# The opening of the convolution stage: nested branches, six PSUM banks, high and low parts first, two stores by SyncE

## The reference

```python
scores = 0.125 * q @ k.T            # 8 heads of 64: window 32, or window 32 with dilation 4
x = softmax(where(mask, scores, -1e9)) @ v
e = argmax(x @ w_gate)              # or the expert before, where sigmoid(x @ w_local) >= 0.5
y = p[e] * (relu(x @ w1[e]) @ w2[e])            # 8 experts, 512 -> 1024 -> 512
gate = sigmoid(sum_k conv_w[k] * y[t - 4 + k])  # 5 taps along the sequence, per channel
out = (gate * (y @ w_val)) @ w_out
```

## Time and profile before

| | before |
|---|---|
| median of 3 runs | 598.66 us (597.76 to 599.15) |
| the profiled execution, its own time | 595.05 us |
| its span in the profile | 593.3 us |
| PE busy | 544.3 us (92%) |
| DVE busy | 267.0 us (45%) |
| ACT busy | 216.0 us (36%) |
| POOL busy | 257.3 us (43%) |
| instruction fetch of PE (queue q8) | 34 packets, 0.56 MB |

### The profile page before, as it was taken

One profiled execution on the slowest core, in us unless ns is written; L12 is line 12 of the kernel. 1 busy time (PEld: TensorE's weight loads), 2 busy tenths in 40 slices (PEclk: granted clock), 3 DMA queues, 4 the chain that ended last, 5 costly groups with the idle time before them and its releaser, 6 DMA issues.

```text
span 593.3 us, 10062 instructions
## 1 busy us (share of the span) xinstructions
PE 544.3 (92%) x3274; PEld 461.8 (78%) x3274; DVE 267.0 (45%) x858; ACT 216.0 (36%) x503; POOL 257.3 (43%) x161
## 2 busy tenths in 40 slices
PE   7899999973779999999999999999899586999997
PEld 3789988862568888888888887888688486999986
DVE  4677777755821121312222121122112689998710
ACT  2677777741021221212212121121112555565421
POOL 1000010471168475937275559674953445621210
PEclk9999999995889999999999999999999589999999
DMA  5849499959079996996889797979681522211012
GB/s 170 248 131 265 106 271 315 285 184 288 21 220 372 327 371 210 373 320 244 269 289 312 256 347 221 398 246 382 230 272 51 148 63 66 90 50 54 36 72 88
DMA packets 62772, 128.42 MB, mean 216 GB/s; under 512 B 9664, under 2 KB 17856, under 8 KB 62208
## 3 DMA queue, kind: packets, MB, share of 16 engines
q1 hardware_dynamic: 38560, 68.43, 35.7%
q0 software_dynamic: 17392, 46.93, 24.6%
q10 hardware_dynamic: 6768, 12.36, 6.0%
HBM read 104.28 MB, written 23.41 MB: 215 GB/s over the span
## 4 chain that ended last, share of the span: by engine, by line
PE 56%; DMA 21%; DVE 8%; POOL 6%; issue 5%; SPq 3%; ACT 1%; PEldq 0%; POOLq 0%; ACTq 0%; DVEq 0%
PE bank L1159 39%; DMA stage<-in_moe_w 10%; PE bank L1176 5%; POOL w_low L564 5%; PE bank L1197 4%; DMA w_high<-in_moe_w 3%; DMA dil_logits<-lg_dil 2%; PE bank L1185 2%; PE bank L1312 2%; DVE gate_acc L971 2%; DMA kT<-in_k 2%; DMA stage<-in_moe_w_val 1%; PE bank L1220 1%; DMA vwin<-in_v 1%; PE bank L1375 1%
## 5 line engine op out<-in xcount | busy, mean ns | idle before, releaser
L564 POOL TENSOR_TENSOR w_low<-stage,w_high 128x2048 fp32r<-128x2048 f32 x32 | 146.8, 4595 | 82.3 <-DMA stage<-in_moe_w 59.0
L1159 PE MATMUL bank<-w_high,x_high 128*128 x184 | 74.7, 406 | 5.7 <-POOL w_low L564 3.1
L1014 ACT ACTIVATE probs<-shifted,negmax 96x128 f32<-96x128 f32 x192 | 66.4, 394 | 35.7 <-PE bank L1185 22.1
L1159 PE MATMUL bank<-w_high,h_high 128*128 x184 | 74.2, 403 | 1.4 <-POOL w_low L564 1.4
L917 DVE TENSOR_TENSOR x_low<-bank,x_high 128x512 fp32r<-128x512 f32 x25 | 17.3, 691 | 127.1 <-ACT x_high L1055 127.1
L1159 PE MATMUL bank<-w_high,x_low 128*128 x184 | 72.6, 394 | 0.0
L1159 PE MATMUL bank<-w_low,x_high 128*128 x184 | 72.1, 392 | 0.0
L1159 PE MATMUL bank<-w_high,h_low 128*128 x184 | 72.1, 392 | 0.0
L1159 PE MATMUL bank<-w_low,h_high 128*128 x184 | 71.7, 390 | 0.0
L1055 ACT CAST x_high<-bank 128x512 fp32r<-128x512 f32 x25 | 14.7, 588 | 152.5 <-PE bank L1283 152.5
L553 POOL DMA_DIRECT2D w_high<-in_moe_w x32 | 24.2, 767 | 101.7 <-DVE x_dil L739 83.4
(11 more groups left out here) (184 smaller groups left out, 1054.5 us busy)
## 6 DMA issues: line engine op xcount, KB each, us to landing
w_high<-in_moe_w POOLq DMA_DIRECT2D x32, 1024.0 KB, 12.8
stage<-in_moe_w SPq DMA_DIRECT2D x32, 1024.0 KB, 7.9
y_sorted<-y_sb ACTq DMA_DIRECT2D x25, 256.0 KB, 7.4
vwin<-in_v SPq DMA_DIRECT2D x4, 1560.0 KB, 7.4
x_sorted<-gathered SPq DMA_DIRECT2D x21, 256.0 KB, 8.2
x_in<-x_sorted ACTq DMA_DIRECT2D x21, 256.0 KB, 5.6
kT<-in_k SPq DMA_DIRECT2D x32, 152.0 KB, 4.7
out<-o_sb SPq DMA_DIRECT2D x18, 256.0 KB, 2.0
```

The lines of the kernel that those rows point to most:

```text
L564: g.tensor_tensor(low, stage[:, c % 2, :], high.bitcast(F32), ALU.subtract).then_inc(split_done, 1)
L1014: a.activation(probs[:, j % 2, u, :], shifted[:, j % 2, u, :], ACT.Exp, bias=negmax[:, j % 2, u:u + 1], scale=-1.0).then_inc(exp_done, 1)
L1159: ins = mm(dst, l, r, start=first and i == 0, stop=last and i == 2)
```

## The change

- PE: the branches past tile 18 are nested. A used tile falls through into the condition of the next one; the first unused tile goes to `pass_unused(first)`, which does in one piece what all remaining steps' `Else` parts did.
- PE: batch 0's six groups go to banks 6, 7, 0, 1, 4, 5, with waits on the expert stage's last readers of those banks, and 6 filler matmuls of 512 columns into bank 2 before the fifth group.
- DVE: the six low parts come first, then three plain copies. ACT: for groups 0 to 2 only the high part, for 3 to 5 the plain copy and the high part.
- ACT waits for `tiles_done` before the group copies and for `pads_ready` only before tap 0. POOL zeroes the pads before the wait for batch 1's rows.
- The stores of the last two tiles are issued by SP between its counting waits.

```diff
         def c_bank(i):
-            return i % 2 + (6 if i < NQ else 0)
+            return (6, 7, 0, 1, 4, 5)[i] if i < NQ else i % 2
         def copied_by(i):
-            return (i - i // 2, i // 2) if i <= NQ else (i - NQ // 2, NQ // 2)
+            return max(i - NQ // 2, 0), min(i, NQ // 2)
...
-            for tile in range(ST):
+            def count_y(tile):
                 sp.wait_ge(y_stored[tile % YB], 16 * (tile // YB + 1))
                 sp.sem_inc(y_count, 1)
+            for tile in range(ST - 3):
+                count_y(tile)
+            for tile in range(ST - 2, ST):
+                sp.wait_ge(y_copied, tile + 1)
+                sp.dma_start(ys_dram[tile * 128:(tile + 1) * 128, :], y_sb[:, tile % YB, :]
+                             ).then_inc(y_stored[tile % YB], 16)
+                count_y(tile - 1)
+            count_y(ST - 1)
...
                 gather_y(t)
+            po.wait_ge(tiles_done, ST + 1)
+            g.memset(cT[:, :, :, 0:PAD], 0.0).then_inc(pads_ready, 1)
             batch_stored(1)
             for t in range(NQ, YR):
                 gather_y(t)
-            po.wait_ge(tiles_done, ST + 1)
-            g.memset(cT[:, :, :, 0:PAD], 0.0).then_inc(pads_ready, 1)
...
             for i in range(NQ):
                 low_c(i)
-                if i % 2 == 1:
-                    plain_c(i)
+            for i in range(NQ // 2):
+                plain_c(i)
...
-                if y_before:
+                if y_before and s < ST:
                     store_y(s - 2)
...
-            store_y(ST - 1)
...
-                if i >= NQ or i % 2 == 0:
+                if i >= NQ // 2:
                     a.copy(cT[:, bb % 2, :, PAD + t * QB:PAD + (t + 1) * QB], src).then_inc(cT_copied, 1)
...
-            act.wait_ge(pads_ready, 1)
+            act.wait_ge(tiles_done, ST + 1)
             for i in range(NQ):
                 high_c(i)
+            act.wait_ge(pads_ready, 1)
             tap0(0)
...
-            for s in range(TOKENS // 128, ST):
-                with pe.If(used > s):
-                    tile_step(s)
-                with pe.Else():
-                    pe.sem_inc(ups_done, 1)
-                    if s + 1 < ST:
-                        pe.wait_ge(xin_split, s + 1)
-                        pe.sem_inc(xin_transposed, 1)
-                    with pe.If(used > s - 1):
-                        for _ in range(10):
-                            mm(bank[:, 6, 0:128], ident[:], ident[:], start=True, stop=True)
-                        down(s - 1)
-                    with pe.Else():
+            def pass_unused(first):
+                pe.sem_inc(ups_done, 1)
+                if first + 1 < ST:
+                    pe.wait_ge(xin_split, first + 1)
+                    pe.sem_inc(xin_transposed, 1)
+                for _ in range(10):
+                    mm(bank[:, 6, 0:128], ident[:], ident[:], start=True, stop=True)
+                down(first - 1)
+                for s in range(first, ST):
+                    if s > first:
+                        pe.sem_inc(ups_done, 1)
+                        if s + 1 < ST:
+                            pe.wait_ge(xin_split, s + 1)
+                            pe.sem_inc(xin_transposed, 1)
                         pe.sem_inc(tiles_done, 1)
                     pe.wait_ge(tiles_done, s + 1)
                     pe.wait_ge(hid_split, 2 * s)
                     pe.sem_inc(hidden_transposed, 2)
-            with pe.If(used > ST - 1):
-                down(ST - 1)
-            with pe.Else():
                 pe.sem_inc(tiles_done, 1)
+            def rest_of_tiles(s):
+                if s == ST:
+                    down(ST - 1)
+                    return
+                with pe.If(used > s):
+                    tile_step(s)
+                    rest_of_tiles(s + 1)
+                with pe.Else():
+                    pass_unused(s)
+            rest_of_tiles(TOKENS // 128)
...
-                if i >= 2:
-                    pe.wait_ge(cT_split, i - 1)
-                    pe.wait_ge(cT_copied, copied_by(i - 1)[0])
-                    pe.wait_ge(cT_copied_v, copied_by(i - 1)[1])
+                if i >= NQ:
+                    free = max(i - 1, NQ)
+                    pe.wait_ge(cT_split, free)
+                    pe.wait_ge(cT_copied, copied_by(free)[0])
+                    pe.wait_ge(cT_copied_v, copied_by(free)[1])
...
+                if n == 1:
+                    pe.wait_ge(cT_copied, copied_by(NQ)[0])
...
-            for i in range(NQ):
-                transpose_rows(i)
+            transpose_rows(0)
+            transpose_rows(1)
+            pe.wait_ge(xin_split, ST)
+            transpose_rows(2)
+            pe.wait_ge(hidden_ready, ST)
+            transpose_rows(3)
             pe.wait_ge(out_weights, 2)
+            keep_clock(wv_high, 6, 2)
+            pe.wait_ge(hid_split, 2 * ST)
+            transpose_rows(4)
             pe.wait_ge(y_copied, ST)
+            transpose_rows(5)
```

## The result

The changed kernel took 599.57 us (median of 20 runs, 594.52 to 607.16), the kernel before 597.56 on the same chips (20 runs, 593.30 to 605.57). The ratio is 1.0057, interval 1.0032 to 1.0081: slower by 3.4 us, between 1.9 and 4.8. The forecast was +4.2 us. The profiled execution took 601.90 us with a span of 600.1.

A forecast was written before the change was run, and what follows sets the result against it. DVE, then PE, bounds the conv stage, so the end follows group 6's low part: T0 471.1 plus 11.4 gives 482.5 against 478.27, 4.2 us later. Median 598.66 + 4.2 = 602.9 us; range 595.5 to 608.0.

The forecast's parts named there:

- The branch at tile 23: PE's branch at tile 23's condition: 3.0 to 5.6 us instead of 0.69, down product ending 0.8 us later.
- The way out of the nest: PE's exit after the last used tile: five jumps, two waiting for instruction fetches, 7.6 us together, bounds 6.0 and 11.2.
- T0: Start of batch 0's first y transposes: forecast at 471.1 us, bounds 469.2 and 477.5, against 464.45 before.
- rival B: Nest exit needs one fetch of 3.0 to 5.6 us; group 6's low part -0.5 to +2.1, likeliest +0.3; chance 0.14.
- the signs of being wrong: Trace signs: five jumps near 0.3 us with transposes before 466, one long jump, or gaps in DVE after group 6.
- A: Rival: nest jumps cheap, five at 0.3 us; low part of group 6 2.6 to 4.5 us faster, taken 3.2; chance 0.22.
- C: Rival: as forecast, but DMA rings full at both fetches and the tile 23 branch; +8 us or more; chance 0.06.
- The opening: From T0 to group 6's low part: 11.4 us instead of 13.8, banks and order giving 2.4 us.
- The steps at nothing: Small parts (pads, ACT's new wait, stores by SP) priced at 0, bounds -0.3 and +1 us.
- Stores by SP: Last y stores moved to SP: y_count 25 within 1 us of before, nothing on the path; price 0.
- Pads first: POOL zeroes pads before gathers 6 and 7, which slip 0.3 to 1 us; cost nothing.
- Behind group 6: After group 6's low part: 23.0 us of DVE work and 91.4 us of PE work, untouched by the change.

The follow-up runs named there:

- c0: The kernel before, unchanged, profiled and timed once more under a second name; 597.29 us against 597.46, ratio 1.0002.
- e2: The changed kernel with the linear branches of the kernel before instead of the nest; 596.27 us against 596.68, ratio 1.0025.
- e10: The changed kernel with the last two stores of y issued by ACT as before; one execution, 600.64 us.
- e3: The kernel before with 10 more fillers in each never-entered Else part, shifting later code; 599.31 us, ratio 1.0044.
- e7: Changed kernel, linear branches, unused steps' releases in a tail, 18 to 22 under one condition; 586.20 us once; again ("e7 again") 593.00 against 597.46, ratio 0.9918.
- e9: e8 without the six filler matmuls of 512 columns in the opening; one execution, 587.26 us against 597.57 for one of before.
- e1: The kernel before with only the nested branches added; 601.33 us against 596.68, ratio 1.0091.
- e8: e7 with DVE's three plain copies moved between the fourth and fifth low part; 590.38 us once, then 594.75 median, ratio 0.9960.

## Why the prediction was right, and where it was wrong

**Sign and size.** Slower was right, and 602.9 lies 3.3 us above the 599.57 measured; 1.1 us of that is the kernel before, which in the long comparison stood at 597.56 and not at 598.66. The other 2.2 are the difference of the medians, 2.0 measured against 4.2. By the ratio it is 3.4 against 4.2. The time alone would have borne the prediction out; the trace doesn't in the step that decides.

**The branch at tile 23: right.** Taken as 3.0 to 5.6 us, it was 3.42, and its price was taken as 0.8: H to E is 8.40 against 7.71, so 0.7 (0.46 of pause, and fillers of 2.47 instead of 2.23). The branch starts at 454.00, q8's packet at 455.02, and the branch ends at 457.42, 1.4 us after the packet.

**The way out of the nest: right that it waits for a fetch, wrong in the count.** This is the step that failed. The prediction read the nest from the source: five `If` blocks close one after another, so five jumps, through the pieces 26, 27, 27, 28, 28 and 29, with two fetches and 7.6 us. The trace has one. By my count of the compiled program every jump at the end of a true side goes straight to one place, instruction 7464, behind the whole nest. The one executed here starts at 6814, so it skips 650 instructions and lands in piece 29. It costs one fetch, and that fetch is dearer than either of the two: 5.01 us, of which 2.6 pass before the packet starts, 0.9 are the packet and 1.5 come after. DMA is 0.77 busy in that stretch. E to T0 is 7.41 us where the steps of the prediction give 10.2, 2.8 less. That the jumps are threaded into one was rival B, at 0.14, and the prediction's own list has one long jump among the signs of being wrong. So what came is B. B's price for the fetch, 3.0 to 5.6, held this one; its likeliest value did not. B put the low part of group 6 at -0.5 to +2.1 us: from H it comes 2.0 us later than in the profile of before and 3.5 later than in c0. A, the cheap jumps, has T0 3.7 us behind E (463.8 against 460.14), and C more than 10.2; both fall with the 7.41. (The upper bound of T0, 477.5, is 477.0 by the prediction's own terms, and +10.6 is +10.1; nothing hangs on it.) The chance that the count was wrong should have been higher, as it hung on the order in which an assembler writes jumps, which no row of the trace of before shows.

**The opening: right in form, 0.65 us too short.** All six groups are transposed without a wait for DVE or ACT, as said: the first four in 2.82 us (2.5 forecast), the fillers in 2.30 (2.6 forecast). PE starts at half the clock and is back at the full one for value(0):

```profile
473.10:475.00 1.90, 1.90 (x12) 1.90 (x13) 0.41 (x1) 0.82 (x2) 0.00 (x0) 0.50 0.65 216
...
478.60:480.60 2.00, 1.90 (x16) 1.66 (x14) 0.92 (x2) 1.61 (x4) 1.39 (x3) 1.00 0.60 182
```

These are rows of the windows view. In DVE's timeline the 2.42 us stall of the earlier trace rows is down to 0.27 ahead of group 6:

```profile
480.71 1.48 DVE L960 COPY cT<-bank 128x384 f32<-128x384 f32 x3
483.19 1.67 DVE L980 SCALAR_TENSOR_TENSOR gate_acc<-cT,convw,gate_acc 128x576 f32<-128x576 f32 x2 [1.01 <-ACT gate_acc L1118]
485.13 0.56 DVE L968 TENSOR_TENSOR cT_low<-bank,cT_high 128x384 fp32r<-128x384 f32 x1 [0.27 <-ACT cT_high L1110]
```

The three copies at 1.48 us are where they were expected. The low part of group 5 starts 7.15 us after T0 and that of group 6 4.90 later: 12.05 against 11.4. The value of this part was overrated for another reason. It was set against 13.82 us, and c0 shows 12.58 for the same code. In that execution the clock came back inside value(0) (granted 0.83 in 470 to 476 us, against 0.56 in 471.6 to 477.0 of the first profile), and DVE's stall was 1.17 us instead of 2.42. So banks and order save 1.8 us against one execution of before and 0.5 against the other; e2 says 1.7 and 0.4. The prediction had written 2.4 from one trace. A term that hangs on the clock in a stretch of 5 us needed a second level beside it, as the fillers were given one. c0's row, to be held against the last of the earlier trace rows:

```profile
475.48 0.56 DVE L959 TENSOR_TENSOR cT_low<-bank,cT_high 128x384 fp32r<-128x384 f32 x1 [1.17 <-issue]
```

**The sum.** Against the profile of before: +0.7 (H to E), +3.0 (E to T0), -1.8 (opening) = +2.0 us, where 4.2 had been written. Against c0: +0.7 +3.3 -0.5 = +3.5 us. The measured 3.4 (1.9 to 4.8) holds both. So that the forecast came near the measurement is in part luck. It has two errors that offset one another: 2.8 us too much for the fetches (2.5 against c0), and 0.6 to 1.9 us too much for the gain in the opening, as one sets it against one or the other trace of before.

**The steps at nothing: right here, and one only under its cover.** Stores by SP: e10 agrees with 0. Pads first: 0 with a T0 as late as here. Before's own order, with T0 4.36 and 4.11 us after E, had 0.30 and 0.03 us to spare. e3 shows the price with T0 2.58 us after E, some 2.3 us of waiting for POOL. It is likely that e7 to e9, with T0 2.4 to 2.7 us after E, rest on the move; none of them was run with the old order of POOL, so this is not shown. Behind group 6: 23.7 and 91.3 us, as said.

**What stays open.** e1 and e2 split the change into +5.4 us (3.5 to 7.4) and +1.5 us (-1.0 to +4.0) by the ratios. Their traces say +3.6 and -1.9 against the profile of before, +5.1 and -0.4 against c0. By c0 the two agree within the intervals, by the other they don't quite. What makes the time ahead of H differ between executions, 449.7 to 462.2 us, was not pursued: the code there is the same in all these kernels. Why the branch at tile 23 became 3.0 us long in e3 is read, not shown: by my count the jump ahead of it enters the piece there, q8's packet starts 0.67 us after that landing, and the target stands five instructions short of the next border. No run takes it apart.

## What to carry to other kernels

Count the places of far branches in the compiled program, not in the source: a branch that skips code costs by which piece of 256 instructions it lands in and by whether the landing runs on into the next, here 0.2 us or 2 to 5, and code that is never executed decides it. Issue a far branch while the engine still has queued work: 2.9 us beneath a down product of 5.5 cost nothing in e7, and of 5.0 us with an empty queue 3.3 showed in the changed kernel. Before a stretch is sped up, look for what its slowest member has covered: here the pads (e3), then the gathers (e9).

## What the runs showed of the hardware that was not expected

- A fetch of instructions has a constant end and a loose beginning. From the end of q8's packet to the end of the branch it is 1.4 to 1.5 us in all nineteen branches over 1.5 us that the fourteen traces have behind 440 us. The packet took 0.88 to 1.54 us. The time from the branch to the packet's start was 1.0 us at 454.0 of the changed kernel (no other packet in flight) and 2.6 at 468.0 (DMA 0.77 busy); that the busy DMA is the reason is not shown.
- Two equal branches can differ by a factor of nine: L1362 took 2002 ns in before and 223 in e3, with the same operands and outcome.
- The rest ahead of the opening doesn't alone decide its clock. After 7.40 us of rest the changed kernel's transposes had 0.50 (a group in 0.64 us). After 2.49 us those of e7 had 1.00 (0.34 us) and the fillers too. After 2.72 us e7 again had 0.91 over the transposes and then 0.50 over the fillers (465.4 to 468.0), with PE never idle between them. e8, with a rest of 2.41 us, shorter than e7's, had 1.00 over its transposes and then 0.53 (462.4 to 464.7). The lower clock, 6.68 against 4.99 us from T0 to the low part of group 5, is nearly all of what sets e7's two openings apart.
